# Which slots hold two weight jobs, and where the attention loads stand in SyncE's queue

## What is computed

```python
def _attn_ref(q, k, v, n_sink, window):          # q, k, v: 2 x 8 x 768 x 64
    scores = scale * np.matmul(q, k.transpose(0, 1, 3, 2))
    keep = is_sink | in_window                   # 4 sinks, 128 keys back
    scores = np.where(keep, scores, -1000000000.0)
    a = np.exp(scores - np.max(scores, axis=-1, keepdims=True))
    a = a / (np.sum(a, axis=-1, keepdims=True) + 1e-09)
    return np.matmul(a, v)

def reference(...):
    x = attn_out as 1536 tokens x 512
    g = x @ w_gate;  x = ((g / (1 + exp(-g))) * (x @ w_val)) @ w_out      # d_ff 1536
    h = x @ w_in;    return (max(h, 0) + alpha * min(h, 0)) @ w_out2      # d_ff 2048
```

## Time and profile before

| | before |
|---|---|
| median of 3 runs | 632.41 us (631.68 to 632.77) |
| the profiled execution's own time | 632.77 us |
| its span, first to last instruction | 631.0 us |
| TensorE busy | 619.7 us, 98% of the span |
| POOL busy | 452.5 us, 72% |
| VectorE busy | 407.8 us, 65% |
| ScalarE busy | 243.8 us, 39% |
| stretch of the head (slots 0 to 19) | about 0 to 39 us |
| stretch with attention slots among MLP chunks (slots 20 to 54) | about 39 to 199 us |

### The profile page before, as it was taken

The page is one execution under the profiler, slowest core; times in us unless marked ns, Lnnn a source line. Parts: engine busy times, 40 slices in busy tenths (PEclk is TensorE's granted clock), DMA queues, the critical chain, the costliest instruction groups (busy, mean ns, idle before and its releaser), DMA issues.

```text
span 631.0 us, 9373 instructions
## 1 busy us (share of the span) xinstructions
PE 619.7 (98%) x3066; PEld 486.9 (77%) x3066; DVE 407.8 (65%) x696; ACT 243.8 (39%) x585; POOL 452.5 (72%) x600
## 2 busy tenths in 40 slices
PE   7989999999999999999999999999999999999997
PEld 4567776776777888888887888887888888888886
DVE  4954667556486956564747474898776567756474
ACT  5635653644545632121213030445535424442150
POOL 6958688877788989998989573689999987810000
PEclk9999999999999999999999999999999999999999
DMA  9443332411223112221212321100222222000004
GB/s 289 124 151 117 127 96 98 125 62 52 83 68 84 34 35 66 68 66 35 67 34 68 100 85 51 48 4 17 68 66 68 68 67 85 17 1 0 2 17 184
DMA packets 29391, 45.67 MB, mean 72 GB/s; under 512 B 2880, under 2 KB 9024, under 8 KB 29344
## 3 DMA queue, kind: packets, MB, share of 16 engines
q1 hardware_dynamic: 29200, 44.81, 23.0%
q10 hardware_dynamic: 144, 0.26, 0.2%
HBM read 41.92 MB, written 3.15 MB: 71 GB/s over the span
## 4 chain that ended last, share of the span: by engine, by line
PE 91%; POOL 2%; DVE 2%; ACT 1%; DMA 1%; issue 1%; SPq 0%; DVEq 0%; ACTq 0%; POOLq 0%
PE ffn_ps L1991 29%; PE att_ps L1966 24%; PE ffn_ps L1906 15%; PE att_ps L1991 8%; PE ffn_ps L1966 6%; PE att_ps L1853 3%; PE att_ps L1817 2%; PE att_ps L1832 2%; DMA raw_weights<-pieces 1%; PE att_ps L1906 1%; POOL scratch L1758 1%; POOL w_lo L1678 1%; PE att_ps L1863 1%; DVE scratch L2220 1%; PE att_ps L1811 0%
## 5 line engine op out<-in xcount | busy, mean ns | idle before, releaser
L1678 POOL TENSOR_TENSOR w_lo<-raw_weights,w_hi 128x512 fp32r<-128x512 f32 (+1 forms) x128 | 155.9, 1218 | 10.3
L1677 POOL CAST w_hi<-raw_weights 128x512 fp32r<-128x512 f32 (+1 forms) x128 | 79.5, 621 | 33.1 <-PE ffn_ps L1991 17.2
L2337 DVE TENSOR_TENSOR scratch<-ffn_ps,scratch 128x512 f32<-128x512 f32 x108 | 73.9, 686 | 34.7 <-PE ffn_ps L1991 34.2
L1706 POOL TENSOR_TENSOR w_lo<-part_sum,w_hi 128x256 fp32r<-128x256 f32 x80 | 59.7, 747 | 6.4
L1906 PE MATMUL ffn_ps<-x_hi,w_hi 128*128 128x512 f32 x152 | 61.7, 406 | 0.7 <-DVE x_lo L2246 0.6
L1906 PE MATMUL ffn_ps<-x_hi,w_lo 128*128 128x512 f32 x152 | 59.4, 391 | 0.0
L1906 PE MATMUL ffn_ps<-x_lo,w_hi 128*128 128x512 f32 x152 | 59.2, 389 | 0.0
L1991 PE MATMUL ffn_ps<-h_hi,w_hi 128*128 128x512 f32 x130 | 51.6, 397 | 0.0
L1991 PE MATMUL ffn_ps<-h_hi,w_lo 128*128 128x512 f32 x130 | 50.7, 390 | 0.0
L1991 PE MATMUL ffn_ps<-h_lo,w_hi 128*128 128x512 f32 x130 | 50.6, 389 | 0.0
L1758 POOL TENSOR_TENSOR scratch<-scratch,inv 128x264 f32<-128x264 f32 (+1 forms) x48 | 30.0, 625 | 28.3 <-DVE inv L2209 28.2
(11 more groups left out here) (208 smaller groups left out, 1572.9 us busy)
## 6 DMA issues: line engine op xcount, KB each, us to landing
raw_weights<-pieces SPq DMA_DIRECT2D x122, 256.0 KB, 2.7
k_sb<-kt SPq DMA_DIRECT2D x12, 264.0 KB, 3.4
v_sb<-vt SPq DMA_DIRECT2D x12, 256.0 KB, 2.7
out<-scratch SPq DMA_DIRECT2D x12, 256.0 KB, 2.0
q_sb<-qt SPq DMA_DIRECT2D x11, 256.0 KB, 3.4
scratch<-vs SPq DMA_DIRECT2D x1, 384.0 KB, 6.9
q_sb<-qt ACTq DMA_DIRECT2D x1, 256.0 KB, 2.6
alpha<-alpha_t SPq DMA_DIRECT2D x1, 8.0 KB, 6.8
```

The costliest lines, as they stand in the source:

```text
L1677: chain(pool.tensor_copy(hi, raw[:, r % n_raw, at]))
L1678: last = pool.tensor_tensor(lo, raw[:, r % n_raw, at], hi.bitcast(F32), ALU.subtract)
L1706: pool.tensor_tensor(lo, s, hi.bitcast(F32), ALU.subtract).then_inc(split_done, 1)
L2337: ins = dve.tensor_tensor(to, back_ps(key), total, ALU.add)
```

## The change

The first edit makes the even slots the ones with two weight jobs, from slot 20 on. The second and third put V c one slot earlier in SyncE's list (before the pieces of slot 4c - 5 rather than 4c - 4), and K c one slot earlier as well (4c - 8 rather than 4c - 7).

```diff
-        for _ in range(1 if n % 2 == 0 or plan[slot_plan[n] + 1][0] == "tsum" else 2):
+        for _ in range(1 if n % 2 or plan[slot_plan[n] + 1][0] == "tsum" else 2):
...
-                if n_pairs * c - 4 <= n and c < n_quads:
+                if n_pairs * c - 5 <= n and c < n_quads:
                     load_values(c)
                     c += 1
-                if n_pairs * c - 7 <= n and n % n_pairs == 1 and c < n_quads and c > RING + 1:
+                if n_pairs * c - 8 <= n and n % n_pairs == 0 and c < n_quads and c > RING + 1:
                     load_keys(c)
```

## The result

The changed kernel takes 649.5 us (median of 5 runs, 648.8 to 651.6) against 632.1 us for the kernel before (median of 5): a ratio of 1.0277, with a 95% interval of 1.0257 to 1.0298. It is slower by 17.4 us. The forecast was 646.0 us in a range of 639.5 to 652. The profiled execution took 650.5 us, with a span of 648.8 us, 17.8 us more than the 631.0 of before.

The account below looks back on a forecast made before the run. TensorE, busy 98% of the span, was taken to set the time. Waits of 3.6, 3.8, 3.2 and 3.0 us add up to 13.6, all other parts zero: 632.41 + 13.6 = 646.0 us, range 639.5 to 652.

Parts of the forecast that it names:

- The mechanism: In SyncE's queue, pieces stuck behind waiting key loads delay POOL's normalisation, so TensorE's turn waits four times, 13.6 us.
- K10: Key load 10 in SyncE's queue: spared, its piece stays a job of slot 35, no wait of TensorE.
- K7: Key load 7 in SyncE's queue, a piece behind it: TensorE waits 3.6 us, turn at 61.73 instead of 58.12.
- K8: Key load 8 in SyncE's queue, a piece behind it: TensorE waits 3.8 us, turn at 81.09 instead of 77.25.
- K9: Key load 9 in SyncE's queue, a piece behind it: TensorE waits 3.2 us, turn at 99.14 instead of 95.90.
- K11: Key load 11 in SyncE's queue, a piece behind it: TensorE waits 3.0 us, turn at 136.70 instead of 133.67.
- the lower bound: All four late pieces land after 2.7 us, as one issued alone: waits together 8.5 us, time 640.9 us.
- the rival: TensorE's clock falls in the four waits, at least 1.3 us each: 651.2, up to 656 us; chance 0.14.
- the first case: Four TensorE waits as summed, without a clock fall: 640.9 to 648.1 us, forecast 646.0; chance 0.68.
- the second case: The four TensorE waits, and its clock falls as well: 648 to 656 us; chance 0.14.
- The rival that was not slower: SyncE's queue does not hold the pieces, so no normalisation is late: 631.6 us; chance of faster 0.02, no change 0.05.
- The rival of only some waits: Some of TensorE's four waits stay hidden; with two of four hidden 639.8 us, case 635 to 641; chance 0.09.

Follow-up runs that it names:

- the run with later loads: New parity, with key and value loads one slot later than in the kernel before: 631.1 us, ratio 0.9995 against the kernel before.
- The filler run: Changed kernel plus 8, 14, 11 and 8 filler matmuls on TensorE ahead of the four waiting turns: 643.7 us, ratio 1.0191 against the kernel before.

## Why the prediction was right, and where it was off

**What bounds the kernel.** Right, though the reading of the waits was not complete: the line of 1.9 us in the earlier trace rows is one of two that name POOL (2.7 us together, all in the head), and TensorE has two waits for ScalarE in the mixed stretch, of 0.4 us each, not one. Neither changes the argument. TensorE had nothing to win back, as the run with later loads shows, and every wait put on it reached the end in full: 18.0 us at 220 us, 17.8 at the end.

**The mechanism.** Right in its place and in its count: four waits, at the turns of units 18, 22, 26 and 34, none at K10, each behind a piece that had moved behind a key load. That both edits are needed was in the argument (the parity puts the late piece ahead of the normalisation, the key edit makes it late), and the runs with one of them gave 0 and 2.0 us. POOL's waits for pieces came to 30.4 us, where 20 or more were forecast. The values edit was put at zero; beside the parity it made 0.4 us, and beside both other edits it added nothing, both within the noise.

**The sum of the waits.** 13.6 us were forecast, 12.3 measured. Term by term: K7 3.6 against 2.66, K8 3.8 against 3.92, K9 3.2 against 3.21, K11 3.0 against 2.50. The error of K7 is its landing and split: P10 was issued at 53.73 and POOL started on it at 57.26, 3.5 us later instead of 4.1, and needed 1.9 us to the normalisation instead of 2.26, because the long subtraction of 1.61 us in the earlier trace rows did not recur. P33, with no other piece queued behind it, was started on 3.4 us after its issue, not 3.8. The value taken from the row behind keys, rather than the 2.7 us of a piece that lands alone, was the right choice: by the lower bound the waits would have been 8.5 us.

By the Trainium skill's price of a transfer (DMA: Bandwidth & Descriptors, "Anatomy of one DMA — SWDGE (gpsimd) path"), a fit to transfers issued by GpSimd where these are issued by SyncE, the waits were to be some 8 us; they were 12.3. From the issue of the four pieces behind keys and queries to POOL's start it took 3.5, 4.6, 3.8 and 3.4 us, more than the 2.6 us that the Trainium skill's price gives as an estimate for a transfer alone.

**The clock: the step that was mis-sized.** The forecast took the case without a fall as the likeliest (0.68) and gave the other 0.14, at 1.3 us or more for each wait, 651.2 us and up to 656. The clock fell after three of the four waits and cost 6.6 us, more than the whole difference between the forecast and the measurement. So the term that the forecast put at nothing measured 6.6 us. The filler run shows that this is the clock and not the waiting itself: the turns are as late, the clock stays up, and the loss is 12.2 us. The price of 1.3 us came from the head of the kernel, where six matmuls were slow; after the waits here 12, 11 and 7 or so were. The argument against the rival, that no row showed a fall, was empty: no row of the kernel before has TensorE idle for more than 1.5 us ahead of work either, so the trace could not have shown one. The measured 649.5 us lies above the first case (640.9 to 648.1) and inside the second (648 to 656). The case that came true, at three of the four waits, is thus the one with a chance of 0.14, and the forecast of 646.0 was only 3.5 us off because the waits came out 1.3 us too high while the 6.6 us were left out; the range caught the result because it had been drawn to hold most of the second case. That closeness is in part luck. With the measured waits and the clock's 6.6 us, the sum would have been 632.1 + 18.9 = 651.0, of which 0.9 us is the head of this execution.

The Trainium skill (TensorE: Matmul & The Clock Gate, "Part 1: The HAM clock gate"), which has half rate as the resting state that idleness brings back, spoke for the rival and was right here: 0.50 from 84 to 88 us after 3.9 us without a matmul. It deserved the larger chance.

**The rival that was not slower**, that SyncE's queue does not hold the pieces, has fallen: with a fifth buffer the same pieces pass ahead of the key loads, and the loss goes.

**The rival of only some waits** has fallen too: all four came, and none was shorter than 2.5 us.

## What to carry to other kernels

In a queue that is worked off in order, a load with an unmet wait delays everything behind it, so ask of each load that moves not when it will land but which instruction stands behind its consumer. Here a piece late by some microseconds cost 2 us at most as long as POOL did the urgent small operation first, and 17 us when two harmless-looking table entries put the piece first. And when a saturated TensorE is made to wait, add the slow matmuls afterwards to the price of the wait: here 6.6 us on top of 12.3. In the three traces without fillers that have such waits, of 2.5 to 3.9 us, the clock fell after eight of nine; in the same traces and in that of before it stayed up after waits of 0.8 us and less.

## What was not expected of the hardware

The length of a wait did not decide alone whether the clock fell: after 2.50 us (unit 34) it fell, after 2.66 us (unit 18) it did not, in the same execution, and in the run without the values edit it fell at unit 18 after 2.63 us. Nor did it always fall within the wait: in that run TensorE had been at work again for some 0.8 to 1 us, at full rate, before the matmuls became slow, at units 18, 22 and 26. The loss does not follow the length either: 1.3 us after a wait of 3.00 us, 1.6 after 3.83 and 2.6 after 3.92. What sets this is open. In single executions the clock also fell without the waits: one of 15 executions of the kernel before had a granted clock of 0.989 and took 636.2 us.
